# A recurrent attention and two MLP layers on one core: the gate kept in PSUM, and five smaller moves around it

## The reference, cut to what matters

```
B, H, S, D = 4, 8, 768, 48          # r, k, v: [B, H, S, D]; w, u: [H, D]
for t in range(S):                   # a recurrence with a state of D x D per head
    y[t]  = r[t] @ (state + (u * k[t]) v[t]^T)
    state = w * state + k[t] v[t]^T
x  = y as [B*S, H*D] = [3072, 384]
h  = x @ w_in    (384 -> 2048);  x = (h * sigmoid(1.702 h)) @ w_out    (2048 -> 384)
h  = x @ w_in2   (384 -> 2048);  out = (h * tanh(softplus(h))) @ w_out2 (2048 -> 384)
```

## Time and profile before

| | |
|---|---|
| median of 3 executions | 891.18 us (891.11 to 891.25) |
| the profiled execution | 891.0 us |
| span of its profile | 889.2 us |
| mean granted clock of TensorE | 0.998 |
| TensorE busy | 882.1 us, 99% |
| VectorE busy | 328.7 us, 37% |
| ScalarE busy | 292.5 us, 33% |
| GpSimd busy | 156.4 us, 18% |

### The profile page before, as it was taken

The page is one execution under the profiler, slowest core; times in us unless marked ns, Lnnn a source line. Parts: engine busy times, 40 slices in busy tenths (PEclk is TensorE's granted clock), DMA queues, the critical chain, the costliest instruction groups (busy, mean ns, idle before and its releaser), DMA issues.

```text
span 889.2 us, 12953 instructions
## 1 busy us (share of the span) xinstructions
PE 882.1 (99%) x5168; PEld 730.6 (82%) x5168; DVE 328.7 (37%) x460; ACT 292.5 (33%) x540; POOL 156.4 (18%) x126
## 2 busy tenths in 40 slices
PE   9999999999999999999999999999999999999998
PEld 8998888887888878878888888888888888888886
DVE  6878336424443443543244222222222221221111
ACT  4542332232223222222454422322322322322322
POOL 5998403322231331120000000000000000000000
PEclk9999999999999999999999999999999999999999
DMA  9554303212330332221430000000000000000000
GB/s 248 170 170 118 95 25 97 83 48 63 88 99 12 86 93 63 51 77 38 157 107 18 1 0 1 36 1 1 35 1 1 36 1 1 35 1 1 36 1 35
DMA packets 37836, 49.54 MB, mean 56 GB/s; under 512 B 5873, under 2 KB 30322, under 8 KB 37778
## 3 DMA queue, kind: packets, MB, share of 16 engines
q1 hardware_dynamic: 37120, 48.13, 18.2%
q10 hardware_dynamic: 658, 0.59, 0.3%
HBM read 36.11 MB, written 4.72 MB: 46 GB/s over the span
## 4 chain that ended last, share of the span: by engine, by line
PE 96%; POOL 1%; DVE 1%; issue 1%; ACT 0%; POOLq 0%; DVEq 0%
PE h L1016 44%; PE acc L1045 43%; PE a_bank L895 2%; PE pair L928 2%; PE pair L941 1%; PE a_bank L953 1%; PE acc L878 1%; POOL win_lo L482 0%; POOL wout_lo L487 0%; DVE g_lo L798 0%; PE pair L878 0%; POOL arena L457 0%; PE h L895 0%; PE pair L914 0%; PE pair L921 0%
## 5 line engine op out<-in xcount | busy, mean ns | idle before, releaser
L798 DVE TENSOR_TENSOR g_lo<-act,g_hi 128x512 fp32r<-128x512 f32 (+1 forms) x202 | 173.1, 858 | 507.0 <-ACT g_hi L592 506.8
L1016 PE MATMUL h<-xs,win_hi 128*128 128x512 f32 (+1 forms) x1212 | 340.6, 384 | 0.2 <-POOL win_lo L482 0.2
L1016 PEld LDWEIGHTS h<-xs,win_hi 128*128 128x128 f32 x1212 | 220.2, 188 | 45.1 <-issue 0.7
L589 ACT ACTIVATE act<-h 128x512 f32<-128x512 f32 (+1 forms) x202 | 116.4, 576 | 268.9 <-PE h L1016 266.0
L592 ACT ACTIVATE g_hi<-h 128x512 fp32r<-128x512 f32 (+1 forms) x202 | 116.5, 577 | 254.4 <-PE acc L1045 254.3
L1045 PE MATMUL acc<-g_hi,wout_hi 128*128 128x512 f32 (+1 forms) x606 | 168.1, 379 | 0.0
L1045 PE MATMUL acc<-g_hi,wout_lo 128*128 128x512 f32 (+1 forms) x606 | 167.8, 379 | 0.0
L1045 PE MATMUL acc<-g_lo,wout_hi 128*128 128x512 f32 (+1 forms) x606 | 167.6, 378 | 0.0
L1016 PE MATMUL h<-xs,win_lo 128*128 128x512 f32 (+1 forms) x606 | 164.8, 380 | 0.0
L1045 PEld LDWEIGHTS acc<-g_hi,wout_hi 128*128 128x128 f32 x606 | 111.6, 189 | 21.8
L1016 PEld LDWEIGHTS h<-xs,win_lo 128*128 128x128 f32 x606 | 111.2, 188 | 22.0
(11 more groups left out here) (92 smaller groups left out, 373.3 us busy)
## 6 DMA issues: line engine op xcount, KB each, us to landing
arena<-in_rk SPq DMA_DIRECT2D x44, 192.0 KB, 3.3
mid<-in_wts SPq DMA_DIRECT2D x16, 384.0 KB, 7.8
arena<-in_wts SPq DMA_DIRECT2D x16, 384.0 KB, 3.5
xs<-xt SPq DMA_DIRECT2D x117, 48.0 KB, 2.0
arena<-in_k SPq DMA_DIRECT2D x22, 192.0 KB, 2.6
arena<-in_r SPq DMA_DIRECT2D x22, 192.0 KB, 3.1
arena<-in_v SPq DMA_DIRECT2D x22, 192.0 KB, 2.7
out<-mid SPq DMA_DIRECT2D x5, 768.0 KB, 3.3
```

The source lines that it names most:

```text
L589: act.activation(act1[:, g % 2, 0:c1 - c0], h_bank[g % 2][:, 0:c1 - c0], GATES[layer])
L798: dve.tensor_tensor(g_lo[:, g % 2, cols], act1[:, g % 2, cols], f32(g_hi[:, g % 2, cols]), ALU.subtract).then_inc(glo_done, 1)
L1016: ins = pe.matmul(hb, w[:, f, kd, :], x_part(lo, par, kd)[:, c0:c1], start=i + kd == 0, stop=i == 2 and kd == KD - 1)
```

## The change

Six edits.

1. The gate is written back into the PSUM bank `h`, in place of `act1` in SBUF. The high part is a copy of it with rounding, behind a wait for the first pass. `split_g` subtracts the high part from the bank. `up(g)` waits for the split of g - 2. `act1` goes; the `amat` of sequence 0 lies in the second buffer of edit 2.
2. `xt` has two buffers, and `x_hi_part(n)` waits for the moves of n - 2 in place of n - 1.
3. The four halves of rk of the sequences 0 and 1 are all issued by SP, in the order of the sequences.
4. `selector_rows` multiplies each head's piece of u by a row of 128 columns of the identity in place of one column; ScalarE copies every 128th column. `WARM` is (4, 6) in place of (5, 10).
5. In tile 0 the diagonal of a sequence is made one step later, behind the next unit's `split_g`.
6. On SP the loads of k, v and r for sequence n + 2 stand ahead of the moves of sequence n, other than for the last sequence of a tile.

```diff
-WARM = (5, 10)
+WARM = (4, 6)
...
-        xt = sb("xt", [P, 2, HP, CH], F32R)
+        xt = sb("xt", [P, 2, 2, HP, CH], F32R)
...
-        act1 = sb("act1", [P, 2, TT])
...
-                e.amat = act1.rearrange("p a t -> p (a t)").rearrange("p (a h t) -> p a h t", a=2, h=HP)
+                e.amat = xt[:, 1].bitcast(F32)
...
+        def h_cols(g):
+
+            f, c0, c1 = unit(g)
+            return h_bank[g % 2][:, 0:c1 - c0]
...
-            return xt[0:PR_ROWS, lo].rearrange("p (a i) t -> p a i t", a=2)
+            return xt[0:PR_ROWS, n % 2, lo].rearrange("p (a i) t -> p a i t", a=2)
...
-                sp.dma_start(buffers(n).rk[0:rk_rows(n)], rk_half(n, 0)).then_inc(rk_in[n % B], 16)
-                if n >= EARLY:
-                    sp.dma_start(buffers(n).rk[ODD:PR_ROWS], rk_half(n, 1)).then_inc(rk_in[n % B], 16)
+                rows = rk_d[bass.ds(n, 1)].rearrange("o j d a h t -> (o j d) a h t")
+                for r0, r1, p0 in ((0, ODD if n < EARLY else D, 0), (D, 2 * D, ODD)):
+                    sp.dma_start(buffers(n).rk[p0:p0 + r1 - r0], rows[r0:r1]).then_inc(rk_in[n % B], 16)
...
                     load_rk(n + 2)
+                    if n % B < B - 1:
+                        load_rest(n + 2)
                 move_x(n)
-                if n + 2 < NT * B:
+                if n + 2 < NT * B and n % B == B - 1:
                     load_rest(n + 2)
...
-                if n > B:
-                    act.wait_ge(moved[(n - 1) % B], moves(n - 1))
+                if n > B + 1:
+                    act.wait_ge(moved[(n - 2) % B], moves(n - 2))
...
                 act.wait_ge(h_done, g + 1)
-                if g >= 2:
-                    act.wait_ge(glo_done, g - 1)
-                act.activation(act1[:, g % 2, 0:c1 - c0], h_bank[g % 2][:, 0:c1 - c0], GATES[layer])
+                act.activation(h_cols(g), h_cols(g), GATES[layer]).then_inc(g_full, 1)
                 if g >= 2:
                     act.wait_ge(g_used, g - 1)
-                act.activation(g_hi[:, g % 2, 0:c1 - c0], h_bank[g % 2][:, 0:c1 - c0], GATES[layer]).then_inc(g_done, 1)
+                act.wait_ge(g_full, g + 1)
+                act.activation(g_hi[:, g % 2, 0:c1 - c0], h_cols(g), ACT.Copy).then_inc(g_done, 1)
...
-            for n in range(EARLY):
-                act.dma_start(first[n].rk[ODD:PR_ROWS], rk_half(n, 1)).then_inc(rk_in[n], 16)
...
-                act.activation(pick[p0:p0 + D, :], decay_bank[p0:p0 + D, 0:HP], ACT.Copy).then_inc(pick_copied, 1)
+                act.activation(pick[p0:p0 + D, :], decay_bank[p0:p0 + D, 0:HP * P:P], ACT.Copy).then_inc(pick_copied, 1)
...
                     select(SCORES[t][s])
+                if t and s in SCORES[t]:
                     diagonal(SCORES[t][s])
+                if t == 0 and s - 1 in SCORES[t]:
+                    diagonal(SCORES[t][s - 1])
...
-                dve.tensor_tensor(g_lo[:, g % 2, cols], act1[:, g % 2, cols], f32(g_hi[:, g % 2, cols]), ALU.subtract).then_inc(glo_done, 1)
+                dve.tensor_tensor(g_lo[:, g % 2, cols], h_cols(g), f32(g_hi[:, g % 2, cols]), ALU.subtract).then_inc(glo_done, 1)
...
-                        ins = pe.matmul(decay_bank[p0:p0 + D, hp:hp + 1], u_row[:, d0:d0 + D], ident[0:1, 0:1], start=True, stop=True)
+                        ins = pe.matmul(decay_bank[p0:p0 + D, hp * P:(hp + 1) * P], u_row[:, d0:d0 + D], ident[0:1, :], start=True, stop=True)
...
                 if g >= 2:
-                    pe.wait_ge(g_done, g - 1)
+                    pe.wait_ge(glo_done, g - 1)
```

More of the change, by code:

```diff
@@ L212, in mlp_rwkv_program @@
         h_done = sem("h_done")
+        g_full = sem("g_full")
         g_done = sem("g_done")
@@ L259, in x_pieces @@
                     q0 = hp % 2 * ODD + done
-                    yield f32(xs[q:q + m, :, par * KD + kd, cols]), f32(xt[q0:q0 + m, :, half * 2 + hp // 2, :])
+                    yield f32(xs[q:q + m, :, par * KD + kd, cols]), f32(xt[q0:q0 + m, n % 2, :, half * 2 + hp // 2, :])
                     done += m
@@ L997, in up @@
                 par = t % 2
-                hb = h_bank[g % 2][:, 0:c1 - c0]
+                hb = h_cols(g)
                 pe.wait_ge(win_ready, layer * NF + f + 1)
                 if g >= 2:
-                    pe.wait_ge(g_done, g - 1)
+                    pe.wait_ge(glo_done, g - 1)
                 if f == 0 and layer:
```

## The result

The changed kernel takes 893.97 us (median of 20 executions, 889.80 to 896.21), the kernel before 890.94 on the same chip (20 executions, 887.75 to 891.73). The ratio is 1.0038 (95% interval 1.0026 to 1.0049): slower by 0.38%, where the prediction said 0.47% faster. The range 885.0 to 889.4 doesn't hold it. What happened is rival D, to which I had given 0.07 and 895.5 us.

The account below looks back on a forecast made before the run. TensorE, 99% busy, was taken as the bound, through its work, waits and clock. 891.0 - 2.0 - 0.2 - 3.2 + 1.1 = 886.7; the runs' median is 0.2 higher, so 886.9, rounded to 887.0 us; range 885.0 to 889.4.

Parts of the forecast that it names:

- rival D: Tile 0's late diagonal becomes the new stall, sequences 2, 3 and 5 costing 1.5 + 1.7 us each: 895.5 us, chance 0.07.
- What bounds the kernel: TensorE, 99% busy: only its work, waits and clock count; one 1.5 us wait for VectorE plus 1.7 us of clock.
- The gate: Split reading PSUM and `g_hi` is never stretched, so sequence 6's state update comes about 5 us earlier: -3.2 us.
- rival C: The wait at 83 us stays, the predicated copy held up in the split's place: 890.2 us, no change, chance 0.12.
- Diagonals a unit later: In tile 0, TensorE stalls 0.5 us at sequence 3, 0.5 to 0.6 at sequence 2, later ones covered: +1.1 us.
- The start: Fewer warming products, dense turning of u and earlier rk bring the first `inside` from 15.50 us 2.0 us earlier.
- B: Start gives little (clock low until 11.4, turn unpaired or rk late): 0.7 in place of 2.0, 888.3 us, chance 0.18.
- -0.2 for the weight half: TensorE's 0.2 us wait at 34 us for a low weight half that GpSimd makes goes away.
- Edits priced at nothing: Two buffers for x out, and loads of k, v and r ahead of the moves, were taken to change no time.

Follow-up runs that it names:

- e10_before_dots_psum: The kernel before with only the predicated copy's data (the eight sums) in PSUM and none of the six edits: 886.53 us, ratio 0.9961.
- e12_dots_gate: The kernel before with the eight sums in PSUM and the gate written back into its PSUM bank: 888.98 us, ratio 0.9982.
- e5_start_alone: The kernel before with only the two start edits (rk all on SP; 128-column turning products with fewer warming products): 889.12 us, ratio 0.9998.
- e4_gate_alone: The kernel before with only the gate in place in PSUM and up's wait on the split: 892.95 us, ratio 1.0022.
- e1_diag_back: The changed kernel with tile 0's diagonal put back right behind the selection: 890.86 us, ratio 1.0005.
- e2_dots_psum: The changed kernel, late diagonal kept, with the predicated copy's data (the eight sums) in PSUM: 887.97 us, ratio 0.9976.
- e6_order_back: The changed kernel with the loads of k, v and r behind the moves of x again: 893.07 us, ratio 1.0032.
- e11_dots_start: The kernel before with the eight sums in PSUM and the two start edits (rk on SP, u's turn with fewer warming products): 888.41 us, ratio 0.9971.
- e3_diag_late: The kernel before with only tile 0's diagonal made a step later, the gate still in SBUF: 894.36 us, ratio 1.0039.
- e8_rk_two_queues: The changed kernel with the second halves of rk issued by ScalarE again: 896.59 us, one execution.

## Why the prediction was wrong, step by step

**"What bounds the kernel": right for the profiled execution.** The 1.5 us wait and its 1.7 us of clock were what there was to gain behind the start. The kernel of e10_before_dots_psum, without them, gains 3.5 us by its ratio, part of which can be its start. But the clock's fall isn't in every execution. Of the 71 of the kernel before in the three sets, 34 have a mean granted clock of 0.998 or less and medians of 891.2 to 891.6 us; the other 37 have 0.999 or more and medians of 889.6 to 889.9. So the 1.7 us were there to gain in about half of the executions, and I had counted them in full from one profile.

**"The gate", -3.2: wrong, and the first of the two steps that failed.** "The form that was never stretched" held in 202 of 202 splits. "Without it the state update is about 5 us earlier and the 3.2 us go" didn't: alone, the edit costs 0.22%. Two things were missed. The copy read two SBUF operands too, stood directly ahead of the split on an engine that works in order, and was held in its stead (4.01 us at 76.16); I had named this as rival C. And I priced `up`'s new wait by a plain unit, where it has 2.5 us to spare. In tile 0 the unit is 256 columns and the split stands behind 3 us of VectorE's other work; there the wait costs 1.7 us even with nothing stretched (e12_dots_gate).

**"Diagonals a unit later", +1.1: wrong, and the step that decides.** Its order term was exact: 0.52 and 0.53 us, measured with the copy in PSUM form. The duration was wrong. I took the median of the earlier trace rows, 1.32 us, and wrote against C, and used for D, that "those copies were stretched by 0.9 us at most". But 16 of those 22 copies stand behind 100 us with no GpSimd instruction beside them. Only the six of tile 0 met GpSimd, at 1.33 to 2.19 us: the median was that of copies left alone, and the longest was that of six chance meetings at the old place, not a bound. The same trait, two operands in SBUF, had been my explanation for a split of 5.48 us a few lines above, and I didn't apply it to the instruction that I was moving onto the path. The real term was 6.0 us of waits and 1.7 of clock, 7.7 in place of 1.1.

**D's mechanism was right, its size nearly, and that in part by luck:** 895.5 against 893.97 us. Its 9.6 us for the diagonals were 1.9 too many, against which the start gave 0.85 less than forecast and the wait for a split came on top with 0.4. I had it fall on sequences 2, 3 and 5 with 1.5 us each, each lowering the clock. It was 0.95, 1.27, 0.28, 2.89 and 0.61 us on sequences 2 to 6, and only the 2.89 lowered it. The Trainium skill's rule ("SBUF — State Buffer", section "Who interferes with whom") pointed to D, and the weight should have gone by it: the trace agrees that an instruction with one operand outside SBUF isn't touched (0.693 us at most in 202 splits). It differs in the length: as I read the rule, VectorE waits for one GpSimd instruction, about 1.0 us here, and the copy was held over four. That section of the Trainium skill says "for the whole instruction" of VectorE's 2-port modes; of two SBUF inputs it says that they contend, and it calls the lock exclusive.

**"The start", -2.0: the direction right in this pair of profiles, the size 1.15.** The turn took 1.88 us (4.03 to 5.91), 1.1 more than before where I had 0.9, and the first scores began at 8.77 (forecast 8.4). The clock was still at the lower level there: the 16 took 1.55 us in place of the 0.9 expected, and only from 10.6 on do the score instructions take the 0.27 us of the higher level, which I had expected by 8.4. rk landed no earlier (decay at 8.81, forecast 8.0), so the second scores weren't early. And by four other profiles most of even the 1.15 isn't the edit's. With the old start the first `up` was at 19.43 us in the profile that I argued from, and at 18.42, 18.77, 18.49 and 18.76 in four kernels with the same code there; the changed kernel's is at 18.27. So against these four the gain is 0.2 to 0.5 us, and B's "the start gives little" was right. Which start is the usual one of the kernel before itself isn't shown, since it has one profile.

**"-0.2 for the weight half": right,** that wait is gone in the changed kernel; it grew where TensorE came early and nothing later held it up (e5_start_alone).

**Edits priced at nothing:** steady units are, as predicted. Edit 6 is worth less than can be told in time, though with it nine copies behind 100 us are stretched. Edit 2 wasn't tried by itself; no wait in the changed kernel names it.

## What to carry to other kernels

When an in-order engine is held up by a neighbour, ask which of its instructions have the trait that gets them held, all of them, and try them one at a time. The one that the profile shows held isn't always the one to free: here the split was held, freeing it passed the hold to the copy ahead of it, and freeing the copy, which looked untouched at that place (1.33 us), took the wait away. A maximum over six meetings at one place is no bound once the instruction is moved, and a median over instructions that met nobody is no price: price a moved instruction by what its form can suffer, and the release of a buffer in the narrowest unit, not the plain one. Compare a change of the start with several executions of the old one, since one profile can be 1 us off by itself.

## What the runs showed of the hardware that I had not expected

**VectorE can be held over several GpSimd instructions.** The copy of 4.32 us above, one of 4.01 (e4_gate_alone) and one of 3.70 us (e1_diag_back): GpSimd's instructions, one right behind the other, run at their full speed of 1.0 us, and VectorE's two-SBUF one, which needs 1.31, ends only as the last of them slows down, to 2.0 us each time. With its data in PSUM the same copy takes 1.33 to 1.40 us in all 110 cases of five kernels, 50 of them beside GpSimd.

**The rise of the clock at the start differs between executions of the same code, by about 2 us of time.** Of e2_dots_psum's eight executions six took 887.93 to 888.31 us and two 890.05 and 890.23; the first of these two is the profiled one, and its rise was late. With the new start the warming products behind the early sums came at 13.26 to 13.47 us in five kernels and at 15.34 to 15.56 in four; the first 16 score instructions took 1.39 to 1.55 us in four of the first group and 2.07 in its fifth (e6_order_back), and 2.08 in all of the second. With the old start, which warms longer, they came at 13.22 to 13.57 in four of five profiles and at 14.23 in the fifth, that of the kernel before. So the shorter `WARM` of edit 4 may make the late rise more frequent; eight of the nine executions of e11_dots_start lie 2 us above its ninth, but that all eight had the late rise is inferred from one profile. By the Trainium skill ("TensorE: Matmul & The Clock Gate", section "What's actually happening"), the number of slow products at the start is run-variable; the profiles agree.

**How long a gap lowers the clock isn't fixed either.** Waits of 1.47 us in the kernel before, 1.58 in e1_diag_back, 1.88 in e4_gate_alone and 2.85 to 2.89 in e3_diag_late, e8_rk_two_queues and the changed kernel were followed by the fall; waits of 1.58 (e6_order_back) and 1.66 us (e5_start_alone) were not. Each fall cost 1.7 us.
